# Fused attention and two feed-forward layers: new places for ScalarE's and VectorE's side work, two joined groups of output products, and second-layer weights loaded one chunk at a time

## What is computed

```python
def sm_attn(qq, kk, vv):
    s = scale * np.matmul(qq, kk.transpose(0, 1, 3, 2))
    a = np.exp(s - max(s)); a = a / (sum(a) + 1e-09)
    return np.matmul(a, vv)
p_packed = sm_attn(p, k, v)
x = sm_attn(q, p_packed, p_packed)          # then to (4608 tokens, 512)
xn = x / sqrt(mean(x*x) + 1e-06) * rms_g
x = (silu(xn @ w_gate) * (xn @ w_val)) @ w_out     # d_ff 1536
h = x @ w_in
out = (max(h, 0) + alpha * min(h, 0)) @ w_out2      # d_ff 2048
```

## Time and profile before

| | |
|---|---|
| runs before | 1567.48, 1569.10, 1569.83 us; median 1569.1 us |
| the profiled execution | 1567.49 us; its span, from the first to the last instruction, 1565.7 us |
| PE busy | 1541.9 us, 98% of the span |
| granted PE clock, mean | 0.998 of full speed |
| DVE, ACT, POOL busy | 45%, 28%, 13% of the span |
| one tile of 24 short blocks with a next batch | 89.4 us (six of them, b = 1 to 6) |

### The profile page before, as it was taken

How to read it: one execution, slowest core, us unless ns; L and a number is a source line. 1 busy time by engine, 2 the same in 40 slices (tenths; PEclk the granted TensorE clock), 3 DMA queues, 4 the chain that set the end, 5 groups by cost and what they waited for, 6 DMA issues and landing times.

```text
span 1565.7 us, 23581 instructions
## 1 busy us (share of the span) xinstructions
PE 1541.9 (98%) x9460; PEld 1263.8 (81%) x9460; DVE 709.3 (45%) x1195; ACT 434.9 (28%) x761; POOL 196.3 (13%) x185
## 2 busy tenths in 40 slices
PE   8999999999999999989999999999999999999999
PEld 3888878787887878779888888888888888888887
DVE  5765655546455555533343333333333333333343
ACT  4445353444444354422211111111111111111111
POOL 2700000000000000062270102020201002020000
PEclk9999999999999999999999999999999999999999
DMA  9312212011121210051220001010000001010000
GB/s 357 104 38 67 65 64 66 32 59 45 64 65 65 66 62 6 5 192 42 99 108 28 27 0 54 0 54 0 33 21 27 27 0 54 0 54 0 26 1 27
DMA packets 53435, 82.35 MB, mean 53 GB/s; under 512 B 16112, under 2 KB 25328, under 8 KB 52976
## 3 DMA queue, kind: packets, MB, share of 16 engines
q1 hardware_dynamic: 48464, 72.37, 13.5%
q10 hardware_dynamic: 4896, 8.92, 1.5%
HBM read 59.25 MB, written 22.02 MB: 52 GB/s over the span
## 4 chain that ended last, share of the span: by engine, by line
PE 89%; ACT 5%; DVE 3%; issue 2%; DMA 1%; POOL 0%; ACTq 0%; DVEq 0%; POOLq 0%
PE psum L665 28%; PE psum L667 27%; PE psum L666 27%; PE psum L801 3%; PE psum L763 1%; DMA rest_mid<-act_sb 1%; ACT act_sb L1144 1%; PE psum L937 1%; PE psum L703 1%; PE psum L718 1%; ACT e L1030 1%; ACT L1092 0%; ACT L1144 0%; ACT L1009 0%; PE psum L751 0%
## 5 line engine op out<-in xcount | busy, mean ns | idle before, releaser
L1477 DVE TENSOR_TENSOR h_lo<-g,h_hi 128x512 fp32r<-128x512 f32 x144 | 105.2, 730 | 472.2 <-ACT h_hi L1184 472.2
L1184 ACT CAST h_hi<-g 128x512 fp32r<-128x512 f32 x144 | 89.4, 621 | 633.7 <-PE psum L667 600.3
L665 PE MATMUL psum<-an_hi,m_hi 128*128 128x288 f32 x768 | 238.5, 311 | 13.9 <-ACT act_sb L1144 12.0
L666 PE MATMUL psum<-an_hi,m_lo 128*128 128x288 f32 x768 | 226.4, 295 | 0.0
L667 PE MATMUL psum<-an_lo,m_hi 128*128 128x288 f32 x768 | 226.3, 295 | 0.0
L665 PE MATMUL psum<-h_hi,ow_hi 128*128 128x512 f32 (+2 forms) x480 | 184.2, 384 | 0.7 <-DVE h_lo L1404 0.7
L665 PEld LDWEIGHTS psum<-an_hi,m_hi 128*128 128x128 f32 x768 | 144.6, 188 | 43.4 <-issue 17.6
L667 PE MATMUL psum<-h_lo,ow_hi 128*128 128x512 f32 (+2 forms) x480 | 177.9, 371 | 0.0
L666 PE MATMUL psum<-h_hi,ow_lo 128*128 128x512 f32 (+2 forms) x480 | 177.4, 370 | 0.0
L1433 DVE TENSOR_TENSOR act_sb<-act_sb,psum 128x288 f32<-128x288 f32 x168 | 75.9, 451 | 165.5 <-PE psum L667 144.8
L666 PEld LDWEIGHTS psum<-an_hi,m_lo 128*128 128x128 f32 x768 | 144.9, 189 | 4.8
(11 more groups left out here) (150 smaller groups left out, 2387.5 us busy)
## 6 DMA issues: line engine op xcount, KB each, us to landing
k_sb<-k_t SPq DMA_DIRECT2D x16, 576.0 KB, 5.2
q_sb<-q_t SPq DMA_DIRECT2D x8, 1152.0 KB, 5.4
xs_raw<-y_mid SPq DMA_DIRECT2D x9, 1024.0 KB, 5.2
out_t<-o_sb ACTq DMA_DIRECT2D x34, 256.0 KB, 2.0
v_sb<-v_s SPq DMA_DIRECT2D x8, 1024.0 KB, 5.6
gv_sb<-w_gv SPq DMA_DIRECT2D x4, 1536.0 KB, 18.7
w_raw_front<-w SPq DMA_DIRECT2D x2, 2560.0 KB, 12.3
y_mid<-y_low SPq DMA_DIRECT2D x7, 512.0 KB, 2.8
```

Of the source, the lines that this page charges most:

```text
L665: nc.tensor.matmul(dst, w_hi, hi, start=start, stop=False)
L666: nc.tensor.matmul(dst, w_lo, hi, start=False, stop=False)
L1184: nc.scalar.copy(h2_hi[:, f % 2, :], g32[:, f % 2, :]).then_inc(g_hi_done, 1)
L1477: nc.vector.tensor_tensor(h2_lo[:, s, :], g32[:, s, :], h2_hi[:, s, :].bitcast(F32), ALU.subtract).then_inc(g_lo_done, 1)
```

## The change

- `fold5` on ACT goes from (between 1) to (after 3), on DVE from (between 1) to (after 4).
- For batches 2 to 7 (tables `LATER`): on ACT the first scores copy stays at (between 0), the second goes to (after 1), both exponentials go from (after 3) to (after 4); on DVE `max0` stays at (between 2), `max1` goes to (after 3), `norm0` and `norm1` go to (within 5). For batch 1 the old places stay.
- `OUT_PIECES`: piece 0 is made after block 4, with piece 1, instead of after block 3; piece 7 after block 11, with piece 8, instead of after block 10. This holds for tiles 1 to 7.
- In tile 7 SP first waits for all three conditions, and then loads the ten front chunks of `w2` one by one (512 KB each): chunk f is issued before `store_rest` of f, once chunk f - 1 has landed. POOL waits for the single chunk.

```diff
 CARRIED = {
     "PE": {(0, "ready", 0): ["fold5_ready"], (0, "after", 0): ["fold5"]},
-    "DVE": {(0, "between", 1): ["fold5"]},
-    "Activation": {(0, "between", 1): ["fold5"]},
+    "DVE": {(0, "after", 4): ["fold5"]},
+    "Activation": {(0, "after", 3): ["fold5"]},
 }
+LATER = {
+    "PE": {},
+    "DVE": {(0, "between", 2): ["max0"], (0, "after", 3): ["max1"], (0, "within", 5): ["norm0", "norm1"]},
+    "Activation": {(0, "between", 0): ["scores0"], (0, "after", 1): ["scores1"], (0, "after", 4): ["exp0", "exp1"]},
+}
+OUT_PIECES = {i: [i - WIDE_LAG] for i in range(WIDE_LAG, 2 * NF1 + WIDE_LAG)}
+for held, joined in ((3, 4), (10, 11)):
+    OUT_PIECES[joined] = OUT_PIECES.pop(held) + OUT_PIECES[joined]
@@ SP, tile 7
-                    load_w2(0, w2_raw_front[:, 0:W2_FRONT // 2, :], 0, W2_FRONT // 2)
                     sp.wait_ge(y_stored, 32 * (BATCH - 1))
-                    load_w2(1, w2_raw_front[:, W2_FRONT // 2:W2_FRONT, :], W2_FRONT // 2, W2_FRONT)
                 for f in range(NF1):
+                    if c == BATCH and f < W2_FRONT:
+                        reached(sp, w2_in[0], 16 * f)
+                        load_w2(0, w2_raw_front[:, f:f + 1, :], f, f + 1)
                     store_rest(b, f)
@@ POOL
-                split_w2(f, w2_in[f // (W2_FRONT // 2)])
+                split_w2(f, w2_in[0], 16 * f + 16)
@@ PE, tile()
-                    if i >= WIDE_LAG:
-                        d, part = (i - WIDE_LAG) // 2, (i - WIDE_LAG) % 2
-                        if i == WIDE_LAG:
+                    for piece in OUT_PIECES.get(i, []):
+                        d, part = piece // 2, piece % 2
+                        if piece == 0:
```

More of the change, by code:

```diff
@@ L56 @@
 DVE_PLACES = {
-    (0, "between", 2): ["max0", "max1"], (0, "between", 3): ["norm0"],
-    (0, "after", 4): ["norm1"], (0, "between", 5): ["turn_a1"], (0, "within", 7): ["packed"],
+    (0, "between", 5): ["turn_a1"], (0, "within", 7): ["packed"],
     (0, "between", 8): ["turn_s0", "gram"], (0, "after", 9): ["shift0"], (0, "between", 9): ["turn_s1"],
@@ L68 @@
 ACT_PLACES = {
-    (0, "between", 0): ["scores"], (0, "after", 3): ["exp0", "exp1"],
     (0, "between", 5): ["turn_a0"], (0, "within", 6): ["turn_a2"],
@@ L89 @@
            (0, "ready", 2): ["scores1_ready"], (0, "after", 2): ["scores1"]},
-    "DVE": {},
-    "Activation": {(0, "between", 1): ["scores0"], (0, "between", 2): ["scores1"]},
[2 rows of a table added]
+}
[3 more added lines that the diff above has]
+    "Activation": {(0, "between", 0): ["scores0"], (0, "after", 1): ["scores1"], (0, "after", 4): ["exp0", "exp1"]},
 }
@@ L349, in build @@
         g_in, alpha_in, p_in, q_in, v_in = map(sem, ("g_in", "alpha_in", "p_in", "q_in", "v_in"))
-        w2_in = [sem(f"w2_in{n}") for n in range(4)]
+        w2_in = [sem(f"w2_in{n}") for n in range(3)]
         k_in = [sem(f"k_in{h}") for h in range(2)]
@@ L408, in at @@
                             beside(c - 1, name)
+                    if 1 < c < BATCH:
+                        for name in LATER[eng.engine.name].get(place, []):
+                            beside(c, name)
                     if c < BATCH:
@@ L539, in _ @@
             sp.wait_ge(y_stored, 32 * NT)
-            load_w2(2, w2_raw_mid[:], W2_FRONT, W2_FRONT + W2_MID)
+            load_w2(1, w2_raw_mid[:], W2_FRONT, W2_FRONT + W2_MID)
             sp.wait_ge(down_mm, H_ALL)
-            load_w2(3, w2_raw_back[:], W2_FRONT + W2_MID, NF2)
+            load_w2(2, w2_raw_back[:], W2_FRONT + W2_MID, NF2)
             sp.wait_ge(x_in, 16)
@@ L633, in _, with split_w2 @@
                 normed(c, 1)
-            def split_w2(f, landed):
+            def split_w2(f, landed, count=16):
                 hi, lo, whole = w2_of(f)
-                pool.wait_ge(landed, 16)
+                pool.wait_ge(landed, count)
                 nc.gpsimd.tensor_copy(hi, whole).then_inc(w2_hi_done, 1)
@@ L650, in _ @@
             for f in range(W2_FRONT):
-                split_w2(f, w2_in[f // (W2_FRONT // 2)])
+                split_w2(f, w2_in[0], 16 * f + 16)
             split_x(0, 0)
             for f in range(W2_FRONT, W2_FRONT + W2_MID):
+                split_w2(f, w2_in[1])
+            for f in range(W2_FRONT + W2_MID, NF2):
                 split_w2(f, w2_in[2])
-            for f in range(W2_FRONT + W2_MID, NF2):
-                split_w2(f, w2_in[3])
             split_x(1, 1)
@@ L899, in tile @@
                              h_lo[:, d % WIDE_SLOTS, :], y_ps, d == 0, d == NF1 - 1, out_mm, down_mm,
-                             lambda: at("ready_down", i))
+                             (lambda: at("ready_down", i)) if piece == OUT_PIECES[i][-1] else None)
                     if i < BLOCKS_OF:
@@ L1067, in beside @@
             def beside(c, name):
-                if name == "scores" and c > 1:
-                    scores_copy(c, 0)
-                    scores_copy(c, 1)
                 if name in ("scores0", "scores1"):
```

## The result

The changed kernel takes 1551.6 us (median of 1550.12, 1551.58 and 1551.79 us) against 1569.1 us. The ratio is 0.9888, with a 95% interval of 0.9865 to 0.9910: 17.5 us less, where 17.8 us had been forecast. On another chip, later, the same kernel took 1549.8 us against 1569.1 us (ratio 0.9881, 0.9865 to 0.9898): 19.3 us less. So the saving is known to about 2 us, and that the first comparison came within 0.3 us of the forecast is in part luck; the last part says why.

What follows compares the result with a forecast made beforehand. PE, busy 98%, was bound by 14 waits for ACT's silu (12.0 us) and time lost around them. Six tiles saving 11.2 us plus tile 7's 6.6 us made 17.8 us: 1569.1 - 17.8 = 1551.3 us, range 1547.5 to 1555.

Steps and rivals of the forecast that it cites:

- Block 3: Tile 5: silu 2 starts at 493.91 and block 3 at 494.38 instead of 495.34.
- Joined blocks 3 and 4: No piece between blocks 3 and 4 costs 0.09 us; block 5 starts at 500.50, its 0.60 us wait gone.
- The chain of the exponentials: Behind silu 4: norm1 ends at 501.76, PE wants turn_a01 at 502.08, 0.3 us to spare.
- The first part: Tile up to block 6: block 6 at about 504.56 instead of 506.15, 1.6 us saved for each tile.
- Blocks 10 and 11: Piece 7 moves behind block 11; the wait before block 13 goes, 0.26 us net a tile.
- Tile 7: Single loads free the first store; block 6 at about 681.2 instead of 686.37; 6.6 us saved in all.
- Later ones fall between two h_lo: Tile 7: later chunks land between two of DVE's h_lo subtractions, said against the rival that POOL holds DVE.
- the rival's 1.7 us: Tile 7: POOL stretches DVE's h_lo and delays a multiplication by 1.7 us, 1553.0 us; chance 0.09.
- The chain's giving back: Chain from silu 4 runs late, turn_a01 and turn_a2 wait, 1.0 us a tile, 1557.3 us; chance 0.14.
- the store's: Tile 7: single loads don't free the store, 5.15 + 1.5 us stay, 1558.0 us; chance 0.08.
- the drain after a table load: Each ACT table load adds about 1.38 us; silu 5 comes 2.8 us later, 1566.3 us; chance 0.02.
- The slower rival: Chain before turn_a01 over 3 us late; at 3.9 us idle PE's clock falls, about 1584 us; chance 0.05.

Runs made afterwards that it cites:

- joined pieces alone: Kernel before with only the `OUT_PIECES` change, tables and loads as before: 1567.0 us, ratio 0.9992.
- places alone: Kernel before with only the new ACT and DVE places (tables), pieces and loads as before: 1563.9 us, ratio 0.9964.
- ten loads at once: Kernel before with the ten chunks loaded by ten single transfers, all issued ahead of the first store of tile 7: 1569.6 us, ratio 1.0005.
- fold5 alone: Kernel before with only `fold5` at its new places (ACT after block 3, DVE after block 4): 1574.6 us, ratio 1.0039.

## Why the prediction was right, point by point

- **What bounds the kernel.** Right: with the 14 waits for silu the time went, and the lines of the account above are the places that were named.
- **Block 3.** Due at 494.38, it came at 489.23 + 5.14 = 494.37; silu 2 at 493.91, as worked out.
- **Joined blocks 3 and 4.** Block 5 at 500.50, it came at 500.47. The joined pieces alone showed that they gain nothing here without the places, and the places alone that silu 4 comes too late without them.
- **The chain of the exponentials.** norm1 at 501.76, it ended at 501.68; turn_a01 at 502.08, it came at 502.04. The spare of 0.3 us was there (0.36 us), and it was enough, since each term was a row of the same operation. The first part gave 1.7 us a tile, not 1.6 (block 6 at 504.44, not 504.56). The rows had this: from block 5 to block 6 it is 4.08 us in the earlier trace rows and the trace of before, 0.11 us of them behind a wait that was to go, so 500.50 + 3.97 = 504.47. The 2.2 us that a tile loses were summed too low as well; the terms beside it (1.35, 0.60 and 0.35 us) make 2.3.
- **Blocks 10 and 11.** The load at 525.2 and the end of silu 12 at 529.9 came as forecast (518.40 and 523.09, plus 5.14 for the start of the tile and 1.7 for the first part); 0.24 us a tile, not 0.26. The joined pieces alone measured about the same, 0.22 us.
- **Tile 7.** Block 6 at 681.2, it came at 672.15 + 9.06 = 681.2 (tile 7 starts 9.06 us earlier). 6.6 us forecast, 6.6 us measured. A load of 512 KB took 3.6 us to land (median of ten, one took 9.9), not 2.8, which cost PE nothing; the stores landed within 3.9 us. That it was the bytes ahead, and not the size of one load, is shown by the ten loads at once.
- **Level of the time.** The saving was taken from the median, 1551.3 us. Taken from the profiled execution it would have been 1549.7 us. Both are times this kernel has (above); which one the median of three falls on is chance, and here two of three were of the slower group. Over all seven executions the median is 1550.1 us.
- **Level of the kernel before.** The prediction had seen that the executions of the kernel before differ and not asked why. Of the 43 later ones (1565.9 to 1571.4 us) 29 had a mean clock of 0.996 or 0.997, with medians of 1569.7 and 1568.6 us, while the traced one had 0.998 and took 1567.5 us. One part of it may be tile 7: behind the stop there the clock stayed at the lower level for 3.4 us in the trace of before, and for about 6.7 us (granted clock 0.50 from 686.4 to 689.7 and from 689.8 to 693.1 us) with the ten loads at once; with the new places alone it was 0.50 from 680.6 to 687.3 us. If so, the change removes that too, which would be why the second comparison saved 19.3 us where the traces account for 18.3. No slow execution of the kernel before was traced, so this stays open.
- **A wrong step that cost nothing.** "Later ones fall between two h_lo": they don't. POOL falls behind, and DVE's subtraction in tile 7 takes 1.4 to 2.5 us in five of six places between 664 and 700 us, the first three of which are:

```profile
666.17 2.52 DVE L1444 TENSOR_TENSOR h_lo<-act_sb,h_hi 128x512 fp32r<-128x512 f32 x1 [0.69 <-ACT h_hi L1159]
...
672.17 1.44 DVE L1444 TENSOR_TENSOR h_lo<-act_sb,h_hi 128x512 fp32r<-128x512 f32 x1 [0.69 <-ACT h_hi L1159]
...
678.09 1.80 DVE L1444 TENSOR_TENSOR h_lo<-act_sb,h_hi 128x512 fp32r<-128x512 f32 x1 [0.69 <-ACT h_hi L1159]
```

In the kernel before, it was three of five between the same times. What saved the rival's 1.7 us is the place: the first stretched one (666.17, block 3) has two pieces behind it, and block 5 follows block 4 after 4.42 us, as in tile 5, where nothing is stretched. That POOL and DVE block each other is what the Trainium skill says ("SBUF — State Buffer", section "Who interferes with whom"), and this trace agrees: POOL's subtraction ran from 665.74 to 668.14, and DVE's ended 0.55 us after it, at 668.69.
- **The rivals.** The chain's giving back was seen where the pieces were not joined (0.7 us a tile); the store's stayed out; the drain after a table load (the Trainium skill, "ScalarE: Activation LUTs", section "What ACT_TABLE_LOAD costs") doesn't show in the changed kernel either: 492.62 + 1.28 us, and the exponential began at 493.92. The slower rival was given too late a start: it counted on the fall of the clock at 3.9 us of idle, the one case in its rows, and 2.35 us were enough in four tiles of six.

## What to carry to other kernels

In a chain of engines with strict queues, moving one step away from a wait can just move the wait: fold5 alone removed the first wait and cost 5.9 us. Walk the next two or three blocks of every queue with durations from the trace, and move the step, what it now stands in front of, and PE's own cover together. A small transfer that somebody waits for should not be issued behind megabytes of others; cut the large ones and put the small one between them. And look at more than one execution before you compare levels: the median of three was as much as 1.5 us off here, while the length of a tile in the trace repeated within 0.05 us.

## What the runs showed of the hardware

- PE fell to its lower clock after a single stop of 2.35 us in four of six otherwise equal tiles, and lost 1.6 us each time (tiles of 91.6 and 90.0 us). A stop of this length has two prices.
- After the same two stops in the opening (1.34 and 1.24 us) the clock came back at 34 us in one execution of the changed kernel and at 38 us in another, 1.9 us apart in the end; with idle matmuls in the stops it was 1.0 in all eight executions, which lie within 1.3 us.
- Ten issues of 512 KB took SP 5.18 us, so many small transfers in a row delay what SP issues behind them.
- A store of 32 KB took 14.58 us to land behind 5 MB of loads in two transfers, 12.18 us behind the same bytes in ten, and at most 3.9 us (median 1.5) where they were issued one at a time between the stores.
